# A linear-attention kernel with two feed-forward layers: the second chunk's y in three banks, weight casts a step later, low parts of x ahead of state sums and half scans

## The reference

```
for t in range(S):                        # B, H, S, D = 2, 8, 768, 48
    cur = einsum('bhd,bhe->bhde', u * k_t, v_t)
    y_t = einsum('bhd,bhde->bhe', r_t, state + cur)
    state = w_t[..., None] * state + einsum('bhd,bhe->bhde', k_t, v_t)
x = y as 1536 tokens x 384
h = x @ w_in                              # 384 x 2048
x = where(h > 0, h, exp(min(h, 0)) - 1) @ w_out      # 2048 x 384
p = probs / (sum(probs) + 1e-9)           # 1536 x 4
for e in range(4):
    out += p[:, e:e+1] * (maximum(x @ w1[e], 0) @ w2[e])   # 384 x 1024, 1024 x 384
```

## Time and profile before

| | |
|---|---|
| median of 3 executions | 660.23 us (660.12 to 660.23) |
| the profiled execution | 660.15 us |
| its span from the first to the last instruction | 658.4 us |
| TensorE busy | 651.6 us |
| VectorE, ScalarE, GpSimd busy | 392.8, 239.6, 244.1 us |
| mean granted TensorE clock | 1.000 of full speed |

### The profile page before, as it was taken

The page is one execution under the profiler, slowest core; times in us unless marked ns, Lnnn a source line. Parts: engine busy times, 40 slices in busy tenths (PEclk is TensorE's granted clock), DMA queues, the critical chain, the costliest instruction groups (busy, mean ns, idle before and its releaser), DMA issues.

```text
span 658.4 us, 12719 instructions
## 1 busy us (share of the span) xinstructions
PE 651.6 (99%) x4687; PEld 599.4 (91%) x4687; DVE 392.8 (60%) x725; ACT 239.6 (36%) x551; POOL 244.1 (37%) x292
## 2 busy tenths in 40 slices
PE   8999999999999999999999999999999999999998
PEld 6999999887788888999999999999999999999997
DVE  7788887756534333656565656565656565656563
ACT  4786655554435444322222222222222222222221
POOL 4897332222031089994008920009910009000000
PEclk9999999999999999999999999999999999999999
DMA  9923223210000033200003200012100011001011
GB/s 327 404 102 120 86 85 123 67 66 2 1 0 1 25 96 97 72 1 1 1 8 106 80 0 1 0 44 100 49 1 0 0 49 49 1 0 48 1 48 49
DMA packets 13279, 38.08 MB, mean 58 GB/s; under 512 B 1968, under 2 KB 4016, under 8 KB 13232
## 3 DMA queue, kind: packets, MB, share of 16 engines
q1 hardware_dynamic: 12944, 37.03, 16.0%
q10 hardware_dynamic: 288, 0.39, 0.2%
HBM read 35.06 MB, written 2.36 MB: 57 GB/s over the span
## 4 chain that ended last, share of the span: by engine, by line
PE 94%; DVE 3%; ACT 1%; issue 1%; DMA 0%; POOL 0%; DVEq 0%; ACTq 0%; POOLq 0%
PE bank L1144 29%; PE bank L1145 29%; PE bank L1146 29%; PE bank L1017 1%; PE bank L1081 1%; PE bank L1093 1%; PE bank L1040 1%; DVE fr L738 1%; PE bank L1070 1%; PE bank L1028 1%; DMA rkw<-rkw_dram 0%; DVE fr L747 0%; DVE att L773 0%; PE bank L1106 0%; PE bank L1103 0%
## 5 line engine op out<-in xcount | busy, mean ns | idle before, releaser
L1144 PE MATMUL bank<-x_lo,w_hi 128*128 128x256 f32 (+2 forms) x432 | 146.2, 338 | 0.7 <-DVE x_lo L808 0.4
L1146 PE MATMUL bank<-x_hi,w_hi 128*128 128x256 f32 (+2 forms) x432 | 143.3, 332 | 0.0
L1145 PE MATMUL bank<-x_hi,w_lo 128*128 128x256 f32 (+2 forms) x432 | 143.1, 331 | 0.0
L1145 PE MATMUL bank<-w_hi,g_lo 128*128 128x384 f32 x384 | 129.6, 338 | 0.0
L1146 PE MATMUL bank<-w_hi,g_hi 128*128 128x384 f32 x384 | 129.3, 337 | 0.0
L1144 PE MATMUL bank<-w_lo,g_hi 128*128 128x384 f32 x384 | 129.0, 336 | 0.0
L691 ACT ACTIVATE g_hi<-bank 128x512 fp32r<-128x512 f32 x96 | 57.5, 599 | 144.2 <-DVE bank L947 122.2
L1144 PEld LDWEIGHTS bank<-x_lo,w_hi 128*128 128x128 f32 x432 | 81.2, 188 | 10.2 <-issue 1.1
L1146 PEld LDWEIGHTS bank<-x_hi,w_hi 128*128 128x128 f32 x432 | 81.2, 188 | 9.0
L1145 PEld LDWEIGHTS bank<-x_hi,w_lo 128*128 128x128 f32 x432 | 81.3, 188 | 8.3
L481 POOL TENSOR_TENSOR raw<-raw 128x128 f32<-128x128 f32 x16 | 7.4, 461 | 200.4 <-DMA raw<-w_dram 200.4
(11 more groups left out here) (111 smaller groups left out, 1149.7 us busy)
## 6 DMA issues: line engine op xcount, KB each, us to landing
raw<-w_dram SPq DMA_DIRECT2D x48, 384.0 KB, 3.6
rkw<-rkw_dram SPq DMA_DIRECT2D x10, 772.5 KB, 4.5
tok<-tok_dram SPq DMA_DIRECT2D x10, 576.0 KB, 5.7
out_dram<-acc SPq DMA_DIRECT2D x10, 192.0 KB, 1.9
rkw<-rkw_dram SPq DMA_DIRECT2D x2, 512.0 KB, 4.3
rkw<-rkw_dram SPq DMA_DIRECT2D x2, 260.5 KB, 3.2
tok<-tok_dram SPq DMA_DIRECT2D x2, 192.0 KB, 5.0
out_dram<-acc ACTq DMA_DIRECT2D x2, 192.0 KB, 2.0
```

Of the source, the lines that this page charges most:

```text
L1144: pe.matmul(out, wh, ml, start=start, stop=False, skip_group_check=shared)
L1145: pe.matmul(out, wl, mh, start=False, stop=False, skip_group_check=shared)
L1146: return pe.matmul(out, wh, mh, start=False, stop=stop, skip_group_check=shared)
```

## The change

TensorE's filler matmuls ahead of the values of chunk 0 go from four to two. The three blocks of chunk 1's y go to banks 4, 3 and 5 instead of all to bank 4; the odd heads' matmuls are issued block by block, with a signal behind each block; ScalarE copies and VectorE subtracts each block at its own signal. ScalarE's half casts of slices 6 to 10 stand a step later in most cases (step 0 has none), and VectorE's low halves of slice 8 as well. At steps 15 and 31 VectorE makes the chunk's low x ahead of `add_update`. At steps 17, 33 and 49 it makes the first block of the low x2 ahead of the half scans, `scale_r` and `lo_g`.

```diff
 NT1 = len(TILES)
+TILE_STARTS = [first // CH for first, _ in TILES]
 STEP1 = NT1 * J1
...
 LO_POOL = (0, 1, 3, 4, 6, 7, 9, 11, 12, 13, 15)
-LO_BETWEEN = {1: (5, 0), 2: (5, 1), 3: (8, 0), 4: (8, 1), 6: (10, 0), 7: (10, 1)}
+LO_BETWEEN = {1: (5, 0), 2: (5, 1), 4: (8, 0), 5: (8, 1), 6: (10, 0), 7: (10, 1)}
 LO_AFTER = {12: (14, 0), 14: (14, 1)}
 STRIP = 32
 STRIPS = DM // STRIP
 PIECES = 4
 HI_FIRST = 6
-HI_BETWEEN = {0: ((6, 0), (6, 1)), 1: ((7, 0),), 2: ((7, 1), (8, 0)), 3: ((8, 1),), 4: ((10, 0),), 5: ((10, 1),),
-              6: ((9, 0), (9, 1)), 7: ((11, 0),), 8: ((11, 1),), 9: ((12, 0), (12, 1)), 10: ((13, 0), (13, 1)),
+HI_BETWEEN = {1: ((6, 0), (6, 1)), 2: ((7, 0),), 3: ((7, 1), (8, 0)), 4: ((8, 1),), 5: ((10, 0),),
+              6: ((10, 1), (9, 0)), 7: ((9, 1), (11, 0)), 8: ((11, 1),), 9: ((12, 0), (12, 1)), 10: ((13, 0), (13, 1)),
               11: ((14, 0), (14, 1)), 12: ((15, 0),), 13: ((15, 1),)}
...
-        BANKS0 = dict(x=bank[6:8], yt=bank[2], kt=bank[5], u=heads_in(bank[6], 0), bonus=bank[3])
-        BANKS1 = dict(x=bank[0:2], yt=bank[4], kt=bank[7], u=heads_in(bank[7], 0), bonus=bank[5])
-        BESIDE = dict(x=bank[6:8], yt=bank[5], kt=bank[5], u=heads_in(bank[7], 256))
+        def blocks_in(b):
+            return [b[:, k * P:(k + 1) * P] for k in range(KT)]
+
+
+        BANKS0 = dict(x=bank[6:8], y=bank[2], yt=blocks_in(bank[2]), kt=bank[5], u=heads_in(bank[6], 0), bonus=bank[3])
+        BANKS1 = dict(x=bank[0:2], yt=[bank[b][:, 0:P] for b in (4, 3, 5)], kt=bank[7], u=heads_in(bank[7], 0),
+                      bonus=bank[5])
+        BESIDE = dict(x=bank[6:8], y=bank[5], yt=blocks_in(bank[5]), kt=bank[5], u=heads_in(bank[7], 256))
...
         s_xh = sem("s_xh")
+        s_y_first = sem("s_y_first")
+        s_xh_first = sem("s_xh_first")
         s_x_first = sem("s_x_first")
...
+
+            def hi_x_block(c, yt, k):
+                if k < KT - 1:
+                    act.wait_ge(s_y_first, k + 1)
+                else:
+                    act.wait_ge(s_py, c + 1)
+                act.copy(x_hi[:, k, chunk(c)], yt[k]).then_inc(s_xh_first if k < KT - 1 else s_xh, 1)
+
...
             hi_w(3)
-            hi_x(0, BANKS0["yt"])
+            hi_x(0, BANKS0["y"])
             hi_w(4)
-            hi_x(1, BANKS1["yt"])
+            for k in range(KT):
+                hi_x_block(1, BANKS1["yt"], k)
             hi_w(5)
...
                 for c in due(n, 3):
-                    hi_x(c, BESIDE["yt"])
+                    hi_x(c, BESIDE["y"])
                 exponential(n)
...
-                dve.wait_ge(s_xh, c + 1)
-                dve.tensor_tensor(x_lo[:, k, chunk(c)], yt[:, k * P:(k + 1) * P], x_hi[:, k, chunk(c)].bitcast(F32),
+                if k < KT - 1:
+                    dve.wait_ge(s_xh_first, k + 1)
+                else:
+                    dve.wait_ge(s_xh, c + 1)
+                dve.tensor_tensor(x_lo[:, k, chunk(c)], yt[k], x_hi[:, k, chunk(c)].bitcast(F32),
                                   ALU.subtract).then_inc(s_x_first if k < KT - 1 else s_x, 1)
...
             mask_scores(1, 1, BANKS1)
-            lo_x(0, BANKS0["yt"])
+            lo_x(0, BANKS0["y"])
             for k in range(KT):
...
                 for c in due(n, 3):
-                    if c < NUPDATE:
+                    if c < NUPDATE and c + 1 not in TILE_STARTS:
                         add_update(c, BESIDE)
-                    lo_x(c, BESIDE["yt"])
+                    lo_x(c, BESIDE["y"])
+                    if c < NUPDATE and c + 1 in TILE_STARTS:
+                        add_update(c, BESIDE)
                 elu(n)
...
                     lo_w(*LO_BETWEEN[n])
+                past = n // J1 - 1
+                if n % J1 == LAG - 1 and n > LAG:
+                    lo_x2(past, blocks_of(past)[0])
                 for part in range(2):
                     for c in due(n, part, HALF_INVERSES):
                         inverses(c, part, 2)
                 for c in due(n, 0, SCALE_R):
                     scale_r(c)
-                past = n // J1 - 1
-                if n % J1 == LAG - 1 and n > LAG and past >= HALF_TILES:
-                    lo_x2(past, 0)
                 lo_g(n)
                 if n % J1 == LAG - 1 and n > LAG:
                     if past < HALF_TILES:
-                        lo_x2(past, 2)
                         lo_x2_both(past)
...
-                rows = slice(b % 4 * STRIP, b % 4 * STRIP + STRIP)
-                return yt[rows, b // 4 * P:b // 4 * P + P]
+                return yt[b // 4][b % 4 * STRIP:b % 4 * STRIP + STRIP, :]
...
                 for k in range(KT):
-                    ins = pe.matmul(yt[:, k * P:(k + 1) * P], bonus_v_sb[:, c % 2, k * P:(k + 1) * P], ident,
-                                    start=first and k == 0, stop=True, is_transpose=first, skip_group_check=True)
+                    ins = pe.matmul(yt[k], bonus_v_sb[:, c % 2, k * P:(k + 1) * P], ident,
+                                    start=first and (k == 0 or c == 1), stop=True, is_transpose=first,
+                                    skip_group_check=True)
                 if not first:
...
-            def values_odd(c, yt, done):
+            def odd_strip(c, yt, b):
+                return pe.matmul(strip_of(yt, b), v_of(c)[:, b * STRIP:(b + 1) * STRIP], att[:, 1, b // 3, :],
+                                 start=False, stop=True, skip_group_check=True)
+
+            def odd_end(c, yt, b):
+                return pe.matmul(strip_of(yt, b), v_odd[:, c % 2, b // 3, :], att[:, 1, b // 3, :],
+                                 start=False, stop=True, skip_group_check=True)
+
+            def values_odd_by_block(c, yt):
                 pe.wait_ge(s_att, c * 2 + 2)
                 pe.wait_ge(s_odd, c + 1)
-                v = v_of(c)
+                odd_strip(c, yt, 2)
+                odd_end(c, yt, 1).then_inc(s_y_first, 1)
+                odd_strip(c, yt, 5)
+                odd_end(c, yt, 4)
+                odd_end(c, yt, 7).then_inc(s_y_first, 1)
+                odd_strip(c, yt, 8)
+                odd_strip(c, yt, 11)
+                odd_end(c, yt, 10).then_inc(s_py, 1)
+
+            def values_odd(c, yt, done):
+
+                pe.wait_ge(s_att, c * 2 + 2)
+                pe.wait_ge(s_odd, c + 1)
                 for p in range(PAIRS):
-                    b = 3 * p + 2
-                    pe.matmul(strip_of(yt, b), v[:, b * STRIP:(b + 1) * STRIP], att[:, 1, p, :],
-                              start=False, stop=True, skip_group_check=True)
+                    odd_strip(c, yt, 3 * p + 2)
                 for p in range(PAIRS):
-                    ins = pe.matmul(strip_of(yt, 3 * p + 1), v_odd[:, c % 2, p, :], att[:, 1, p, :],
-                                    start=False, stop=True, skip_group_check=True)
+                    ins = odd_end(c, yt, 3 * p + 1)
                 ins.then_inc(done, 1)
...
             bonus(0, BANKS0)
-            fill(3, 1)
+            fill(1, 1)
             fill(1, 2)
...
             values_even(1, BANKS1["yt"])
-            values_odd(1, BANKS1["yt"], s_py)
+            values_odd_by_block(1, BANKS1["yt"])
             update(0, BANKS0)
```

## The result

The changed kernel takes 658.75 us (median of 13, 658.66 to 658.77) against 660.22 (13, 660.09 to 660.29): 1.47 us less, ratio 0.9978 with a 95% interval from 0.9969 to 0.9986. The profiled execution took 658.71 us with a span of 656.9, 1.5 less than before.

What follows compares the result with a forecast made beforehand. TensorE, busy 99% of the span, was taken as the bound. GpSimd's 0.5 us, 0.53 at up(16) and 0.68 at down1(16) summed to 1.7 off 660.23: 658.5 us, range 657.8 to 659.3.

Steps and rivals of the forecast that it cites:

- rival (b): GpSimd's row of work ends where it did, so the head gives nothing: 1.2 us less, 659.0; chance 0.22.
- part 5: Steps 17, 33, 49: low x2 ahead of the half scan removes down1(16)'s wait, 0.68 us; nothing at 33 and 49.
- part 4: Steps 15 and 31: low x ahead of the state sum removes up(16)'s wait, the whole 0.53 us.
- Parts 1 to 3: Fewer fills, y by blocks, later casts: up(0) near 18.05, down1(0) about 1.0 us earlier, PE near 0.8 ahead by down1(4).
- Where the gain stops: At up(9) and chunk 3's bonus GpSimd holds PE, so the early 0.8 to 1.0 us is lost but for GpSimd's gain.
- 0.5 (POOL): GpSimd ends slice 9's first low half 0.5 us earlier, near 38.45, by meeting VectorE less; bounds 0 and 1.0.
- The two places of the prediction: GpSimd's subtraction pair at 18.73 ends some 0.2 us earlier; the last product of the pair at 35.84 gains 0.3.
- nothing that I find takes it back by 55.63: GpSimd's 0.5 us gain at slice 9 was to last until its chunk 3 bonus product, which ended at 55.63 before.
- (... and VectorE with it): At up(16), PE wants low x at 61.62, earlier by the head's remaining gain, and VectorE is earlier too.
- (d): Another wait replaces one at up(16) or down1(16), VectorE being late: 0.5 to 1.0 us less, 659.2 to 659.7; chance 0.11.
- (e): Slower: GpSimd meets VectorE's full scans worse at chunk 3's bonus, 0.9 us each; 660.8 with two; chance 0.03.
- (c): The head's gain is kept, GpSimd gaining 1.0 us or not holding up(9): 2.2 less, 658.0; chance 0.12.

Runs made afterwards that it cites:

- the head: Changed kernel with VectorE's reorderings of low x and low x2 undone, leaving fewer fills, y by blocks and later casts: 659.61 us against 660.15 before.
- the two runs with GpSimd's work changed: Changed kernel with one unused 192-column product more on GpSimd, 659.34 us; changed kernel with slice 9's low part moved from GpSimd to VectorE, 657.79 us.
- Part 4 alone: Kernel before the change with only the low x of chunks 3 and 7 put ahead of the state sum: 660.24 us against 660.17.
- the kernel with slice 9 moved: Changed kernel with slice 9's low part moved from GpSimd to VectorE: 657.79 us against 660.15 before.
- the blocks alone: Kernel before the change with only chunk 1's y copied and subtracted block by block: 659.74 us, a single execution.
- the casts alone: Kernel before the change with only the weight casts a step later: 660.18 us, a single execution.
- parts 4 and 5 without the head: Kernel before the change with only low x ahead of the state sum and low x2's first block ahead of the half scans: 658.94 us against 660.15.
- the fills alone: Kernel before the change with only two filler matmuls fewer: 660.01 us, a single execution.
- the added product: Changed kernel with one more 192-column product on GpSimd, result unused, ahead of its low part of slice 9: 659.34 us against 660.15 before.

## Why the prediction was right, and where it was not

The total: forecast 1.7 us less, measured 1.47, inside the range and between the forecast and rival (b). That it came so near is in part luck: as the runs split it, the head gives 0.54, part 5 on top of it 0.91 and part 4 then 0.02, where the sum had 0.5, 0.68 and 0.53.

- **Parts 1 to 3** came as worked out: up(0) at 17.98 (18.05 forecast), down1(0) 1.02 earlier (1.0), the lead at down1(4) 0.77 (0.8; 31.36 against 32.13).
- **Where the gain stops** was right in mechanism: GpSimd holds PE at up(9), and the two runs with GpSimd's work changed show it. The term that was mis-sized is "0.5 (POOL)": GpSimd's low part of slice 9 ended at 38.66, not near 38.45, 0.33 earlier than before, and PE's lead at chunk 3's bonus measured 0.22 to 0.24. The two places of the prediction did give: the pair at 18.8 took 1.67 instead of 1.90, and the last product of chunk 2's terms was met by nothing (the pair took 1.47 instead of 1.93). But other meetings moved too. By the third quarter of slice 7 GpSimd was 0.52 ahead (32.18 against 32.70); its last two quarters then took 1.94 instead of 1.29, more than all of that. The last one had begun 0.10 ahead of VectorE's scaling of k before (33.39 and 33.49) and began 0.06 behind it after (33.04 and 32.98): before, VectorE was held (1.04) and GpSimd was not (0.60), after, VectorE took 0.69 and GpSimd 1.08. Nor did "nothing that I find takes it back by 55.63" hold: of 0.33 there was 0.22 left.
- **Part 4**: the 0.53 appears in the trace (0.24 of lead became 0.75 at up(16)), but not as part 4's. Its parenthesis "(... and VectorE with it)" held the answer and was not followed: VectorE was 0.84 earlier at step 15 by the head alone, so the wait goes in either order. Part 4 alone gives nothing, and its removal costs nothing. It pays with part 5 and without the head (1.21 against 0.66).
- **Part 5**: 0.68 forecast, 0.66 alone. "Just met" was 0.3 in hand: the low x2 ended at 69.09, the load came at 69.42.
- Of the rivals, (b) was nearest on GpSimd's side; (d) and (e) had no part in the whole, though (d) is what part 4 alone does. (c) is about what the kernel with slice 9 moved does (2.2 forecast, 2.36 measured).

Why does the head bring VectorE 0.84 ahead at step 15 when PE is 0.24 to 0.27 ahead? The traces show where it happens, at step 12, where VectorE's first low half of slice 14 meets a quarter of GpSimd's slice 13; first before, then after:

```profile
52.44 0.59 POOL L469 TENSOR_TENSOR w_lo<-raw,w_hi 128x192 fp32r<-128x192 f32 x1
52.49 0.95 DVE L815 TENSOR_TENSOR w_lo<-raw,w_hi 128x384 fp32r<-128x384 f32 x1
```

```profile
52.12 0.55 DVE L834 TENSOR_TENSOR w_lo<-raw,w_hi 128x384 fp32r<-128x384 f32 x1
52.15 0.97 POOL L477 TENSOR_TENSOR w_lo<-raw,w_hi 128x192 fp32r<-128x192 f32 x1
```

Before, GpSimd was first by 0.05 and VectorE was held; after, VectorE is first by 0.03 and GpSimd is held. VectorE's half begins 0.37 earlier and ends 0.77 earlier. All fourteen traces here fit: where the half took 0.91 to 0.99, VectorE reached step 15 as much ahead of the kernel before as it had begun that half; where it took 0.55 or 0.56, 0.4 more (to 0.05). The head alone, the blocks alone and the casts alone are of the second kind, parts 4 and 5 without the head and the fills alone of the first. With the blocks alone PE was only 0.15 ahead at down1(12), and the wait at up(16) was gone all the same. What stays open is the proof by a run: none moves this one meeting and nothing else.

## What to carry to other kernels

A lead won early is worth only what the next engine in a row of its own leaves of it. Before adding up removed waits, look for an engine that has no idle time between the place and the end, even if the list of waits doesn't name it: compare the end of its operation with the load that needs it, and see whether the chain runs through it. Two waits on one busy engine, one behind the other, don't add: removing the first alone lengthens the second by as much. And work moved to another engine pays when it goes into a measured idle stretch (VectorE's 1.33 us at step 7: 0.89 won) and costs when it goes into a full one (step 5: 0.75 lost again).

## What the runs showed of the hardware

The distance from GpSimd's end to the load that waits for it is not the same everywhere: its half of slice 9 ended at 38.66 and up(9) loaded at 38.77, with the added product 39.25 and 39.37, both 0.11 to 0.12 behind; chunk 3's bonus was turned 0.05 behind GpSimd's end. And GpSimd's time for the same work depends on when it meets VectorE by more than expected: chunk 3's bonus product took 1.76 before and 0.83 after, a quarter of a slice 0.59 to 1.45 us in the changed kernel, with no change to GpSimd's own order.

What decides a meeting in these traces is who began first, by a few hundredths of a microsecond, and the one that is held ends at a steady distance behind the other. Four GpSimd operations of 192 columns in a row, from 33.94 on in the kernel before, each met a two-input VectorE operation that had begun earlier, and ended 0.45 to 0.47 behind its end. VectorE's half of slice 14 ended 0.41 behind GpSimd's quarter in the kernel before (53.44 and 53.03). Between the two kernels a shift of 0.37 us turned that meeting round: VectorE's operation took 0.40 less and GpSimd's 0.38 more.
